# Attention scores in two matmul passes instead of three, with stacked query halves and doubled keys

## The chip, the cores and the metric

The kernel runs on one core of one Trainium2 chip. The metric is the device time of one execution in microseconds (us), lower is better. The engines are PE (TensorE), DVE (VectorE), ACT (ScalarE), POOL (GpSimd) and SP (SyncE, which here only issues transfers).

## The reference

Sliding-window attention with four sink tokens, then two mixer layers. Shapes: q, k, v are 2 x 8 x 768 x 64 in fp32; the model width is 512.

```python
scores = q @ k.T / sqrt(64)                # per batch and head
keep = (pos_k < 4) | ((pos_q - pos_k >= 0) & (pos_q - pos_k < 128))
a = softmax(where(keep, scores, -1e9))
x = concat_heads(a @ v)                    # 2 x 768 x 512

h = x.transpose(0, 2, 1) @ U @ V           # mixer 1, rank 32
u = x + h.transpose(0, 2, 1)
x = u + relu(u @ w_ch1) @ w_ch2            # 512 -> 2048 -> 512

h = relu(x.transpose(0, 2, 1) @ w_tok1) @ w_tok2    # mixer 2, 256
u = x + h.transpose(0, 2, 1)
out = u + relu(u @ w_ch1b) @ w_ch2b        # 512 -> 1536 -> 512
```

## The kernel before, in words

Every fp32 product is made of fp32r matmuls on operands that are split in a high part (a cast) and a low part (the value less its high part): high x high, high x low, low x high. So a score is three passes.

Attention works on 12 tiles of 128 queries (T = 0 to 5 are batch 0, T = 6 to 11 batch 1) and, inside a tile, on 8 heads; one head of one tile is a unit u = 8T + h. A head is 64 deep, so two heads (a pair) share the 128 contraction rows: q_hi and q_lo hold a pair in one 128 x 128 block, the even head in rows 0 to 63 and the odd one in rows 64 to 127. To keep the other head out, the key arrays k_hi and k_lo exist once for each head of the pair (index e) with zeros in the rows of the other head; they are set to zero once at the start. Each has three slots of 132 columns: 128 keys of a tile and 4 sink columns. A score matmul reads two slots, 264 columns, and runs over all 128 rows (L841 to L843).

The preparation of tile T + 1 happens during tile T: four PE transposes each for q and k into a bank (L827), an ACT copy out to q_full and k_full (L604, L611; both lie in the array uT_full), a DVE cast to the high part (q: L695, k: two casts of 64 rows, L711, and at T = 0 and 6 two small ones for the sinks, L710), and a POOL subtraction for the low part (q: L346, k: L357, in two steps of 64 rows). For T = 0 DVE does the subtractions. After the scores of a unit, DVE adds the mask and takes the maximum (L727), ACT makes the exponentials (L622), POOL copies the sink columns (L556), PE transposes them two units later (L850), ACT or DVE copies that out, and PE multiplies with v four units after the scores (L869). At the end of a tile (in unit h = 4 of the next one) DVE scales the result to x_nat (L749, L751, L754), and PE takes it in after unit h = 5 (the step "down", L887).

A hand-written list, plan, sets the order on every engine: each engine walks it and does its part of each step, in order, waiting on semaphores. attention(b) writes the units. Batch 0 is attention alone; the units of batch 1 are put one by one between the matmul steps of mixer 1 for batch 0; the rest is mixers alone. SP walks the same list and issues all loads on one queue: q and k of tile T + 2 when the k transposes of T are done, v of the next tile, weights four chunks deep. The helper functions keys, key_parts, query_low, key_low and keys_split and the steps "qsplit", "ksplit" and "scores" are what the change touches.

## Time and profile before

| | |
|---|---|
| median of 3 runs | 672.23 us (671.92 to 672.86) |
| profiled execution, span | 671.3 us |
| PE busy | 651.1 us, 97% |
| POOL busy | 372.9 us, 56% |
| ACT busy | 296.1 us, 44% |
| DVE busy | 204.9 us, 31% |
| share of the 16 DMA engines | 40.4% |

The span is one execution in the profiler, from its first to its last instruction; the median is of other executions, and lies 0.9 us above the span (what is outside the span, and what differs between executions; the profile doesn't part them). Busy shares are means over stages that have different limits: batch 0 of the attention (the first 75 us or so), attention and mixer 1 interleaved (83 to 250 us), and mixers alone. To be read are the stages, the waits of PE in each, and the order in time around the places that the change touches.

### The profile page before, as it was taken

To read this page: it belongs to the slowest core of one execution; us is meant where nothing else is said; L and a number is where in the kernel's file an instruction comes from. 1 tells how busy PE (TensorE), PEld (TensorE's weight loads), DVE (VectorE), ACT (ScalarE), POOL (GpSimd) and SP (SyncE) were. 2 spreads that over 40 slices of the span, in tenths; PEclk is the share of its full clock that TensorE was granted. 3 is DMA by queue.
4 is the path that set the end of the run, shared out by engine and by line. 5 is a ranking of instruction groups with operands and counts; after the bars stand their busy time and mean duration, and the time that the engine had idled before them with its cause. 6 is when DMAs were issued, how large, how long until landed. Compare 5 with 4: busy or idle time off the path is not lost.

```text
span 671.3 us, 10346 instructions
## 1 busy us (share of the span) xinstructions
PE 651.1 (97%) x3652; PEld 587.5 (88%) x3652; DVE 204.9 (31%) x526; ACT 296.1 (44%) x693; POOL 372.9 (56%) x393
## 2 busy tenths in 40 slices
PE   6889999999999999999999999999999999999998
PEld 5878798989999899899999988999999989999996
DVE  7776552333353331231121123111311134012112
ACT  4656565445464444373333324333433347233331
POOL 8544466646555545545665653666666654566562
PEclk9999899999999999999999999999999999999999
DMA  8334254352323333424445442544444442444541
GB/s 182 90 80 111 48 142 125 97 133 79 103 83 91 95 83 106 122 77 116 126 126 172 125 126 59 160 126 127 116 124 128 123 123 80 117 128 126 163 125 63
DMA packets 119955, 76.00 MB, mean 113 GB/s; under 512 B 43968, under 2 KB 103872, under 8 KB 119904
## 3 DMA queue, kind: packets, MB, share of 16 engines
q1 hardware_dynamic: 119904, 75.34, 40.4%
q8 instruction: 30, 0.49, 0.3%
q14 instruction: 21, 0.17, 0.1%
HBM read 71.91 MB, written 3.15 MB: 112 GB/s over the span
## 4 chain that ended last, share of the span: by engine, by line
PE 91%; DVE 4%; issue 2%; ACT 1%; POOL 1%; DMA 0%; DVEq 0%; ACTq 0%; POOLq 0%
PE bank L959 35%; PE bank L984 35%; PE bank L842 4%; PE bank L869 4%; PE bank L850 3%; PE bank L943 3%; PE bank L906 2%; PE bank L887 2%; PE bank L827 1%; PE bank L924 1%; PE bank L980 1%; DVE k_hi L711 1%; DVE masked L727 1%; DVE x_nat L754 1%; DVE sums_eps L749 1%
## 5 line engine op out<-in xcount | busy, mean ns | idle before, releaser
L575 POOL TENSOR_TENSOR w_lo<-w_raw,w_hi 128x512 fp32r<-128x512 f32 (+1 forms) x238 | 301.8, 1286 | 202.1 <-ACT w_hi L596 201.7
L672 DVE SCALAR_TENSOR_TENSOR hid_lo<-bank,hid_hi 128x384 fp32r<-128x384 f32 x112 | 62.4, 558 | 351.9 <-ACT hid_hi L584 351.9
L584 ACT ACTIVATE hid_hi<-bank 128x384 fp32r<-128x384 f32 x112 | 55.0, 491 | 246.5 <-PE bank L959 246.4
L959 PE MATMUL bank<-uT_hi,w_hi 128*128 128x384 f32 x448 | 153.1, 342 | 0.0
L959 PE MATMUL bank<-uT_hi,w_lo 128*128 128x384 f32 x448 | 151.1, 337 | 0.0
L959 PE MATMUL bank<-uT_lo,w_hi 128*128 128x384 f32 x448 | 150.6, 336 | 0.0
L596 ACT ACTIVATE w_hi<-w_raw 128x512 fp32r<-128x512 f32 (+1 forms) x238 | 138.1, 618 | 1.2 <-PE bank L906 1.2
L984 PE MATMUL bank<-w_hi,hid_hi 128*128 128x512 f32 x336 | 134.1, 399 | 0.0
L984 PE MATMUL bank<-w_hi,hid_lo 128*128 128x512 f32 x336 | 132.7, 395 | 0.0
L984 PE MATMUL bank<-w_lo,hid_hi 128*128 128x512 f32 x336 | 132.3, 394 | 0.0
L959 PEld LDWEIGHTS bank<-uT_hi,w_hi 128*128 128x128 f32 x448 | 84.3, 188 | 3.7 <-DVE uT_lo L675 0.2
L959 PEld LDWEIGHTS bank<-uT_lo,w_hi 128*128 128x128 f32 x448 | 84.2, 188 | 3.5
L959 PEld LDWEIGHTS bank<-uT_hi,w_lo 128*128 128x128 f32 x448 | 84.1, 188 | 0.0
L622 ACT ACTIVATE probs<-masked,neg_max 128x264 f32<-128x264 f32 x96 | 49.5, 516 | 74.7 <-DVE neg_max L727 74.2
L984 PEld LDWEIGHTS bank<-w_hi,hid_lo 128*128 128x128 f32 x336 | 63.0, 188 | 13.8
L984 PEld LDWEIGHTS bank<-w_lo,hid_hi 128*128 128x128 f32 x336 | 63.3, 188 | 10.4
L984 PEld LDWEIGHTS bank<-w_hi,hid_hi 128*128 128x128 f32 x336 | 63.3, 188 | 9.6
L556 POOL COPY p_sink<-probs 128x12 f32<-128x12 f32 x96 | 19.0, 200 | 71.2 <-ACT probs L622 69.7
L727 DVE CUSTOM_DVE_ANT_0 masked<-bank,masks 128x264 f32<-128x264 f32 x96 | 41.2, 430 | 40.7 <-PE bank L842 36.8
L869 PE MATMUL bank<-v_nat,probs_T 128*128 128x64 f32 x352 | 50.2, 261 | 0.8 <-DVE probs_T L738 0.4
L869 PEld LDWEIGHTS bank<-v_nat,probs_T 128*128 128x128 f32 x352 | 48.2, 191 | 2.3 <-ACT probs_T L630 1.2
L850 PE MATMUL bank<-ident,probs 128*128 128x128 f32 x176 | 36.2, 280 | 3.9 <-DVE p_sinkT L743 1.7
(82 smaller groups left out, 628.5 us busy)
## 6 DMA issues: line engine op xcount, KB each, us to landing
w_raw<-in_moe_w_ch_dram SPq DMA_DIRECT2D x224, 256.0 KB, 2.8
q_nat<-in_q_dram SPq DMA_DIRECT2D x12, 256.0 KB, 3.0
k_nat<-in_k_dram SPq DMA_DIRECT2D x12, 256.0 KB, 3.6
v_nat<-in_v_dram SPq DMA_DIRECT2D x12, 256.0 KB, 3.2
out_dram<-o_stage SPq DMA_DIRECT2D x12, 256.0 KB, 3.3
w_raw<-in_moe_w_tok_dram SPq DMA_DIRECT2D x6, 256.0 KB, 2.9
w_raw<-in_moe_w_tok_dram SPq DMA_DIRECT2D x8, 192.0 KB, 2.3
U_sb<-in_moe_U_dram SPq DMA_DIRECT2D x3, 96.0 KB, 3.3
```

The source lines that it names most:

```text
L575: nc.gpsimd.tensor_tensor(w_lo[:, split % NW, 0:n], w_raw[:, split % NR, 0:n], w_hi[:, split % NW, 0:n].bitcast(f32), ALU.subtract) \
L584: nc.scalar.activation(dst, m_tile(key)[0:rows, 0:dst.shape[-1]], func).then_inc(hi_ready, 1)
L596: nc.scalar.activation(w_hi[:, split % NW, 0:n], w_raw[:, split % NR, 0:n], ACT.Copy) \
L622: nc.scalar.activation(probs[:, u % 4, :], masked[:, u % 3, :], ACT.Exp, bias=neg_max[:, u % (2 * H):u % (2 * H) + 1], scale=-1.0, accum_o ...
L672: nc.vector.scalar_tensor_tensor(out=dst, in0=src, scalar=0.0, in1=hi.bitcast(f32), op0=ALU.max, op1=ALU.subtract).then_inc(m_drained, 1)
L727: nc.vector.tensor_tensor_reduce(out=masked[:, u % 3, :], in0=s_slots(u)[0][:, 0:NK], in1=masks[:, mask_of(T), :], scale=1.0, scalar=3.0e3 ...
L842: last = mm(bank[:, 0:NK], qs[:, T % 2, h // 2, :], keys(ks, T, h // 2, h % 2), start=(n == 0), stop=(n == 2))
L850: last = nc.tensor.transpose(tp_banks[tp_bank_of[s]][:, j * P:(j + 1) * P], probs[:, u % 4, col:col + P], ident[:, :])
L869: last = mm(o_bank(T)[:, h * D:(h + 1) * D], probs_T[:, u % 2, j * P:(j + 1) * P], v_nat[:, tile % 3, h * D:(h + 1) * D], start=(h == 0 an ...
L943: last = mm(m_tile(use)[:, 0:HALF], tok[:, g, rows], w[:, slot, 0:HALF], start=False, stop=(g == KG - 1 and n == 2), skip_group_check=True)
L959: last = mm(m_tile(use)[:, 0:HALF], w[:, slot, rows], u[:, kk, cols], start=(n == 0), stop=(n == 3 * KD - 1))
L984: last = mm(m_tile(use)[:, :], hid[:, hid_slot(s), toks], w[:, slot, :], start=False, stop=(final and n == 2), skip_group_check=True)
```

## The change

The two scores passes that share the keys' high part become one: for the even head the 128 contraction rows now hold the high part of q in rows 0 to 63 and its low part in rows 64 to 127, and the keys' high part stands in both halves. One pass over it gives high x high + low x high. The second pass has the keys' low part in both halves, and gives high x low and, new, low x low. The odd head is the mirror of this. q_hi and q_lo become one array q_st (index e for the head of the pair); q_lo and the new key_lo are scratch places in uT_full.

Since engines work lane by lane, a low part that was made in rows 0 to 63 comes to rows 64 to 127 by a DMA within the chip. For each tile there are 2 such copies for q and 6 for k, of 64 partitions x 4 x 512 B (128 KB) each; at T = 0 and T = 6 four more for the sinks, 64 partitions x 12 x 16 B each. T = 0 issues them on ACT's queue, the others on SP's, at a new step "stack" that the plan puts at unit h = 4 (for T = 6 behind the last unit of batch 0). PE's first scores of a tile wait for all of them (q_stacked, k_stacked). The casts on DVE now write both copies at once (128 x 1024 where 128 x 512 and 2 x 64 x 512 were), POOL's low part of k is one step of 128 rows where two of 64 rows were. The steps move too: the k transposes and the split of q in batch 0 from h = 2 to h = 1, the split of k from h = 4 and h = 6 to h = 2. Only slot 2 of the key arrays is set to zero at the start.

```diff
             if u == 0:
-                now += [("qT", T), ("kT", T), ("qsplit", T), ("ksplit", T)]
+                now += [("qT", T), ("kT", T), ("qsplit", T), ("ksplit", T), ("stack", T)]
             if lo <= u - LAG_V < hi and (u - LAG_V) % H == H - 1:
                 now.append(("sinksT", (u - LAG_V) // H))
             if u == hi and T < NTILES:
                 now.append(("ksplit", T))
             if u == hi + 1 and T < NTILES:
-                now.append(("ksplit_odd", T))
+                now.append(("stack", T))
             if u < hi and T + 1 < NTILES:
                 if h == 0:
                     now.append(("qT", T + 1))
-                if h == (2, 1)[b]:
+                if h == 1:
                     now += [("kT", T + 1), ("qsplit", T + 1)]
+                if h == 2 and T + 1 < hi // H:
+                    now.append(("ksplit", T + 1))
                 if h == 4 and T + 1 < hi // H:
-                    now.append(("ksplit", T + 1))
-                if h == 6 and T + 1 < hi // H:
-                    now.append(("ksplit_odd", T + 1))
+                    now.append(("stack", T + 1))
...
-        q_hi = sb("q_hi", [P, 2, PAIRS, P], f32r)
-        q_lo = sb("q_lo", [P, 2, PAIRS, P], f32r)
-        k_hi = sb("k_hi", [P, PAIRS, 2, 3, BLK], f32r)
-        k_lo = sb("k_lo", [P, PAIRS, 2, 3, BLK], f32r)
+        q_st = sb("q_st", [P, 2, 2, PAIRS, P], f32r)
+        k_hi = sb("k_hi", [P, 2, PAIRS, 3, BLK], f32r)
+        k_lo = sb("k_lo", [P, 2, PAIRS, 3, BLK], f32r)
...
+        q_lo = uT_full[:, :, 2 * P:3 * P].bitcast(f32r)
+        key_lo = uT_full[:, :, 3 * P:4 * P].bitcast(f32r)
...
+            eng.tensor_tensor(q_lo[:, :, :], q_full, q_st[:, T % 2, 0, :, :].bitcast(f32),
+                              ALU.subtract).then_inc(q_split, 1)
...
+        def key_low_parts(eng, T):
+            eng.tensor_tensor(key_lo[:, :, :], k_full, k_hi[:, 0, :, T % 3, 0:P].bitcast(f32),
+                              ALU.subtract).then_inc(k_split, 1)
+            if T % NQ == 0:
+                for e in range(2):
+                    eng.tensor_tensor(sink_columns(k_lo, e), sink_source(), sink_columns(k_hi, e).bitcast(f32),
+                                      ALU.subtract).then_inc(k_split, 1)
...
+        def stack_queries(queue, T):
+            queue.wait_ge(q_split, T + 1)
+            for rows, other, e in ((TOP, LOW, 0), (LOW, TOP, 1)):
+                queue.dma_start(q_st[other, T % 2, e, :, :].bitcast(f32), q_lo[rows, :, :].bitcast(f32)) \
+                     .then_inc(q_stacked[T % 2], 16)
+        def stack_keys(queue, T):
+            queue.wait_ge(k_split, keys_split(T))
+            slot, done = T % 3, k_stacked[T % 2]
+            for rows, other, e in ((TOP, LOW, 0), (LOW, TOP, 1)):
+                queue.dma_start(k_hi[other, e, :, slot, 0:P].bitcast(f32), k_hi[rows, e, :, slot, 0:P].bitcast(f32)) \
+                     .then_inc(done, 16)
+                for to in (rows, other):
+                    queue.dma_start(k_lo[to, e, :, slot, 0:P].bitcast(f32), key_lo[rows, :, :].bitcast(f32)) \
+                         .then_inc(done, 16)
+                if T % NQ == 0:
+                    for k_pad in (k_hi, k_lo):
+                        queue.dma_start(sink_columns(k_pad, e)[other].rearrange("p a s k -> p (a s) k").bitcast(f32),
+                                        sink_columns(k_pad, e)[rows].rearrange("p a s k -> p (a s) k").bitcast(f32)).then_inc(done, 16)
...
+                elif s[0] == "stack" and s[1]:
+                    stack_queries(sp, s[1])
+                    stack_keys(sp, s[1])
...
-                    pool.wait_ge(q_high, s[1] + 1)
-                    query_low(nc.gpsimd, s[1])
-                elif s[0] in ("ksplit", "ksplit_odd") and s[1]:
-                    pool.wait_ge(k_high, s[1] + 1)
-                    pool.wait_ge(psink_ready, copied)
-                    pool.wait_ge(q_split, s[1] + 1)
-                    if split:
-                        pool.wait_ge(wlo_ready, split)
-                    key_low(nc.gpsimd, pool.wait_ge, s[1], int(s[0] == "ksplit_odd"))
+                    T = s[1]
+                    pool.wait_ge(q_high, T + 1)
+                    pool.wait_ge(q_stacked[(T - 1) % 2], 32 * ((T - 1) // 2 + 1))
+                    query_low(nc.gpsimd, T)
+                elif s[0] == "ksplit" and s[1]:
+                    T = s[1]
+                    pool.wait_ge(k_high, T + 1)
+                    pool.wait_ge(k_stacked[(T - 1) % 2], keys_stacked(T - 1))
+                    key_low_parts(nc.gpsimd, T)
...
+                if s == ("stack", 0):
+                    stack_queries(nc.scalar, 0)
+                    stack_keys(nc.scalar, 0)
...
-                    nc.vector.tensor_copy(q_hi[:, T % 2, :, :], q_full).then_inc(q_high, 1)
+                    nc.vector.tensor_copy(q_st[:, T % 2, :, :, :], q_full.unsqueeze(1).broadcast_to([P, 2, PAIRS, P])) \
+                      .then_inc(q_high, 1)
...
-                    for src, dst, sinks, sink_dst in key_parts(k_hi, T):
-                        if T % NQ == 0:
-                            nc.vector.tensor_copy(sink_dst, sinks)
-                        last = nc.vector.tensor_copy(dst, src)
-                    last.then_inc(k_high, 1)
+                    if T % NQ == 0:
+                        for e in range(2):
+                            nc.vector.tensor_copy(sink_columns(k_hi, e), sink_source())
+                    nc.vector.tensor_copy(k_hi[:, :, :, T % 3, 0:P],
+                                          k_full.unsqueeze(1).broadcast_to([P, 2, PAIRS, P])).then_inc(k_high, 1)
...
-                        pe.wait_ge(q_split, T + 1)
-                        pe.wait_ge(k_split, keys_split(T) - (2 if T % NQ == 0 else 1))
-                    elif h == 1:
-                        pe.wait_ge(k_split, keys_split(T))
+                        pe.wait_ge(q_stacked[T % 2], 32 * (T // 2 + 1))
+                        pe.wait_ge(k_stacked[T % 2], keys_stacked(T))
                     bank, n = s_slots(u)
                     if u >= n:
                         pe.wait_ge(masked_ready, u - n + 1)
-                    for n, (qs, ks) in enumerate(((q_hi, k_hi), (q_hi, k_lo), (q_lo, k_hi))):
-                        last = mm(bank[:, 0:NK], qs[:, T % 2, h // 2, :], keys(ks, T, h // 2, h % 2),
-                                  start=(n == 0), stop=(n == 2))
+                    for n, ks in enumerate((k_hi, k_lo)):
+                        last = mm(bank[:, 0:NK], q_st[:, T % 2, h % 2, h // 2, :], keys(ks, T, h // 2, h % 2),
+                                  start=(n == 0), stop=(n == 1))
```

How the order moves on SP, from the 12th of its rows on (loads of tiles 2 and 3, then of tile 4). Before:

```order
L431 DMA q_nat<-in_q_dram 128x8x64
L433 DMA k_nat<-in_k_dram 128x8x64
L431 DMA q_nat<-in_q_dram 128x8x64
L433 DMA k_nat<-in_k_dram 128x8x64
L439 DMA v_nat<-in_v_dram 128x8x64
```

With the change:

```order
L462 DMA q_nat<-in_q_dram 128x8x64
L464 DMA k_nat<-in_k_dram 128x8x64
L378 DMA q_st<-uT_full 64x4x128 x2
L386 DMA k_hi<-k_hi 64x4x128
L389 DMA k_lo<-uT_full 64x4x128 x2
L386 DMA k_hi<-k_hi 64x4x128
L389 DMA k_lo<-uT_full 64x4x128 x2
```

The eight copies of a tile stand behind the loads of q and k (for two tiles on) in the same queue, and ahead of the load of v.

On ACT at the start of the program, with the change (q_full and k_full are in uT_full; before, nothing stood between the second copy-out and the third):

```order
L646 ACTIVATE uT_full<-bank0 128x4x128 [waits tp_ready]
L378 DMA q_st<-uT_full 64x4x128 [waits q_split]
L378 DMA q_st<-uT_full 64x4x128
L386 DMA k_hi<-k_hi 64x4x128 [waits k_split]
L389 DMA k_lo<-uT_full 64x4x128 x2
L393 DMA k_hi<-k_hi 64x12x4
L393 DMA k_lo<-k_lo 64x12x4
L386 DMA k_hi<-k_hi 64x4x128
L389 DMA k_lo<-uT_full 64x4x128 x2
L393 DMA k_hi<-k_hi 64x12x4
L393 DMA k_lo<-k_lo 64x12x4
L639 ACTIVATE uT_full<-bank4 128x4x128 [waits tp_ready,q_split]
```

ACT's own work for tile 1 now stands behind twelve issues, ten of which wait for the last subtraction of tile 0.

On DVE in a tile of batch 0, from unit h = 1 to the end of tile work in unit h = 4 (L727 and L762 are the masks, two rows each). Before:

```order
L695 CAST q_hi<-uT_full 128x512
L727 ISA masked,neg_max<-bank,masks 128x264
L727 ISA neg_max 128x1
L738 COPY probs_T<-bank 128x256
L743 TENSOR_TENSOR p_sinkT<-bank,p_sinkT 32x128
L727 ISA masked,neg_max<-bank,masks 128x264
L727 ISA neg_max 128x1
L711 CAST k_hi<-uT_full 64x4x128 x2
L727 ISA masked,neg_max<-bank,masks 128x264
L727 ISA neg_max 128x1
L749 TENSOR_SCALAR sums_eps<-sums 128x8
```

With the change:

```order
L730 CAST q_st<-uT_full 128x1024
L762 ISA masked,neg_max<-bank,masks 128x264
L762 ISA neg_max 128x1
L747 CAST k_hi<-uT_full 128x8x128
L762 ISA masked,neg_max<-bank,masks 128x264
L762 ISA neg_max 128x1
L773 COPY probs_T<-bank 128x256
L778 TENSOR_TENSOR p_sinkT<-bank,p_sinkT 32x128
L762 ISA masked,neg_max<-bank,masks 128x264
L762 ISA neg_max 128x1
L762 ISA masked,neg_max<-bank,masks 128x264
L762 ISA neg_max 128x1
```

The casts of k leave the place right ahead of the tile's end work (L749), and stand one unit behind the cast of q.

## Rows read from the trace of the kernel before

**Rows 1.** The page: busy time by engine, chain that ended last.
```profile
PE 651.1 (97%) x3652; PEld 587.5 (88%) x3652; DVE 204.9 (31%) x526; ACT 296.1 (44%) x693; POOL 372.9 (56%) x393
...
PE 91%; DVE 4%; issue 2%; ACT 1%; POOL 1%; DMA 0%; DVEq 0%; ACTq 0%; POOLq 0%
```

**Rows 2.** Stretch of batch 1: length, busy PE, PEld, DVE, ACT, POOL, PEclk, DMA, GB/s.
```profile
83.00:250.00 167.00, 163.94 (x1011) 151.27 (x1010) 62.32 (x192) 85.78 (x222) 97.41 (x117) 1.00 0.37 103
```

**Rows 3.** Timeline of PE, one unit: start, duration, line, names.
```profile
41.21 0.37 PE L842 MATMUL bank<-k_hi,q_hi 128*128 128x264 f32 x1
41.41 0.29 PE L842 MATMUL bank<-k_lo,q_hi 128*128 128x264 f32 x1
41.54 0.28 PE L842 MATMUL bank<-k_hi,q_lo 128*128 128x264 f32 x1
41.66 0.56 PE L869 MATMUL bank<-v_nat,probs_T 128*128 128x64 f32 x4
```

**Rows 4.** Timeline around the end of tile work, in tiles 2 and 5.
```profile
34.66 1.27 POOL L357 TENSOR_TENSOR k_lo<-uT_full,k_hi 64x512 fp32r<-64x512 f32 x1
...
34.79 1.18 DVE L749 TENSOR_SCALAR sums_eps<-sums 128x8 f32<-128x8 f32 x1
...
36.98 1.10 PE L887 MATMUL bank<-x_nat,U_sb 128*96 128x512 f32 x2 [1.35 <-DVE x_nat L754]
...
70.36 0.17 DVE L749 TENSOR_SCALAR sums_eps<-sums 128x8 f32<-128x8 f32 x1
```

**Rows 5.** Timeline of the program's start, up to the first scores.
```profile
5.97 0.60 ACT L611 ACTIVATE uT_full<-bank 128x512 f32<-128x512 f32 x1 [0.26 <-PE bank L827]
...
6.31 0.69 DVE L346 TENSOR_TENSOR q_lo<-uT_full,q_hi 128x512 fp32r<-128x512 f32 x1
...
7.99 1.78 DVE L357 TENSOR_TENSOR k_lo<-uT_full,k_hi 64x48 fp32r<-64x48 f32 x4
...
9.07 0.56 PE L842 MATMUL bank<-k_hi,q_hi 128*128 128x264 f32 x1 [0.93 <-DVE k_lo L357]
```

**Rows 6.** SP's queue: issues in time (start, duration, tile, count).
```profile
3.83 1.08 SPq L433 DMA_DIRECT2D k_nat<-in_k_dram  x1
...
8.49 1.85 SPq L469 DMA_DIRECT2D U_sb<-in_moe_U_dram  x3
...
10.38 1.26 SPq L473 DMA_DIRECT2D o_stage<-o_stage  x2
...
42.91 0.37 SPq L431 DMA_DIRECT2D q_nat<-in_q_dram  x1
```

**Rows 7.** The page's DMA issues: count, KB of each, median us to landing.
```profile
w_raw<-in_moe_w_tok_dram SPq DMA_DIRECT2D x8, 192.0 KB, 2.3
...
o_stage<-o_stage SPq DMA_DIRECT2D x2, 128.0 KB, 3.1
```

**Rows 8.** Groups by form: count, busy us, mean ns, idle before.
```profile
L357 POOL TENSOR_TENSOR k_lo<-uT_full,k_hi 64x512 fp32r<-64x512 f32 x22 | 28.4, 1291 | 7.7 <-DVE k_hi L711 4.2 <-POOL w_lo L575 1.5 <-POOL p_sink L556 0.3
...
L682 DVE CAST v_sink<-o_stage 96x1024 fp32r<-96x1024 f32 x1 | 0.7, 726 | 0.0
L710 DVE CAST k_hi<-uT_full 64x48 fp32r<-64x48 f32 x4 | 0.7, 179 | 0.0
L357 POOL TENSOR_TENSOR k_lo<-uT_full,k_hi 64x48 fp32r<-64x48 f32 x2 | 0.5, 268 | 0.3 <-POOL k_lo L357 0.2
```

**Rows 9.** Timeline of PE: first scores of tiles 1 and 5, last unit of 5, first of 6.
```profile
17.11 0.37 PE L842 MATMUL bank<-k_hi,q_hi 128*128 128x264 f32 x1
...
64.71 0.37 PE L842 MATMUL bank<-k_hi,q_hi 128*128 128x264 f32 x1
...
73.40 0.37 PE L842 MATMUL bank<-k_hi,q_hi 128*128 128x264 f32 x1
...
83.82 0.37 PE L842 MATMUL bank<-k_hi,q_hi 128*128 128x264 f32 x1
```

**Rows 10.** Timeline of DVE: last cast of the keys of tile 6.
```profile
75.03 0.42 DVE L711 CAST k_hi<-uT_full 64x512 fp32r<-64x512 f32 x1
```

More of the change, by code:

```diff
@@ L287, in attention_then_two_mixers @@
         k_split = sem("k_split")
+        q_stacked = [sem(f"q_stacked{i}") for i in range(2)]
+        k_stacked = [sem(f"k_stacked{i}") for i in range(2)]
         probsT_by_act = sem("probsT_by_act")
@@ L344, in query_low @@
         def query_low(eng, T):
-            eng.tensor_tensor(q_lo[:, T % 2, :, :], q_full,
-                              q_hi[:, T % 2, :, :].bitcast(f32), ALU.subtract).then_inc(q_split, 1)
-        def key_low(eng, wait, T, e):
-            low, high = list(key_parts(k_lo, T))[e], list(key_parts(k_hi, T))[e]
-            steps = ((3, 2), (1, 0)) if T % NQ == 0 else ((1, 0),)
-            done = (keys_split(T - 1) if T else 0) + e * len(steps)
-            for to, of in steps:
-                wait(k_split, done)
-                eng.tensor_tensor(low[to], low[of], high[to].bitcast(f32), ALU.subtract).then_inc(k_split, 1)
-                done += 1
-            wait(k_split, done)
@@ L361, in keys_split, with sink_columns, sink_source @@
-        def keys_split(T):
-            return sum(4 if t % NQ == 0 else 2 for t in range(T + 1))
+            eng.tensor_tensor(q_lo[:, :, :], q_full, q_st[:, T % 2, 0, :, :].bitcast(f32),
+                              ALU.subtract).then_inc(q_split, 1)
+        def sink_columns(k_pad, e):
+            return k_pad[:, e, :, :, P:BLK]
+        def sink_source():
+            return k_full[:, :, 0:N_SINK].unsqueeze(2).broadcast_to([P, PAIRS, 3, N_SINK])
+        def key_low_parts(eng, T):
[5 more added lines that the diff above has]
+                                      ALU.subtract).then_inc(k_split, 1)
@@ new lines, in keys_split, with key_moves, keys_stacked @@
+        def keys_split(T):
+            return sum(3 if t % NQ == 0 else 1 for t in range(T + 1))
+        def key_moves(T):
+            return 10 if T % NQ == 0 else 6
+        def keys_stacked(T):
+            return sum(16 * key_moves(t) for t in range(T % 2, T + 1, 2))
+        def stack_queries(queue, T):
[3 more added lines that the diff above has]
+                     .then_inc(q_stacked[T % 2], 16)
@@ L663, in _ @@
         def _(dve):
[L664 to L666 removed]
+            nc.vector.memset(k_hi[:, :, :, 2, :].rearrange("p a b k -> p (a b) k").bitcast(f32), 0.0) \
+              .then_inc(khi_zeroed, 1)
             def low_of(key, rows, dst, hi, relu=False):
```

39 lines of the change are left out of this document (14 added, 25 removed).

## The prediction

> **What bounds the kernel now.** I read the page first, then the stretches, then the waits and the order in time on PE. The page shows PE busy 97% of the span and 91% of the chain that ended last [rows 1]: what leaves PE's stream is gained, where PE really is the last to come. In the stretch of batch 1 it is: PE is busy 163.9 of 167 us there, and the DMA engines at 0.37 [rows 2]. In batch 0 it is so inside a tile: the three score matmuls follow one another without a gap [rows 3]; but once a tile PE waits 1.35 us for x_nat [rows 4]. Before 9.07 us PE has nothing to multiply: the scores of tile 0 wait for its splits [rows 5]. So there are three stages with three limits, and the change touches each in another way.
>
> **What the pass is worth.** In a unit the second pass starts 0.20 us after the first, the third 0.13 us after it, and the next work 0.12 us after that [rows 3]. The third one goes: 0.12 us for each of 96 units. The 48 units of batch 1 give 48 x 0.12 = 5.8 us, since PE is full there and a tile's copies have the time of four units spread over mixer steps. Tile 5, whose successor's copies don't stand between its own units, gives 8 x 0.12 = 1.0 us.
>
> **What the copies cost by themselves.** No row shows a 64-row copy within the chip. The nearest is the copy o_stage<-o_stage: on-chip, also 128 KB, two of them issued in 1.26 us, so 0.63 us each [rows 6], and landed 3.1 us after the issue [rows 7]. The low end is a queue with nothing in the way, 0.37 us for an issue [rows 6] and 2.3 us to landing (192 KB, rows 7); the high end a queue full of loads, 1.08 us for an issue [rows 6]. I take 0.63 and 3.1, the same kind and size.
>
> **The start, tile 0.** The q cast becomes 1024 columns wide; the row of a 1024-column cast says 0.73 us [rows 8]. The cast in use takes 0.2 us less, so the subtraction of q ends at 6.31 + 0.69 + 0.2 = 7.2 us [rows 5]. Behind it on DVE: two sink casts of 0.18, the k cast of 0.73, the subtraction of 0.69, two small ones of about 0.26 each [rows 5, 8]. That is 9.5 us, where it now ends at 9.77 [rows 5]: DVE gains a little. But then ten copies are issued on ACT: the last at 9.5 + 9 x 0.63 = 15.2, landed at 18.3. First scores at 18.3 and not 9.07: **+9.2 us**. Nothing covers this, the whole program waits. ACT's work for tile 1 stands behind these issues too, but PE, DVE and POOL would have nothing for it to feed. Ends: 9.5 + 9 x 0.37 + 2.3 = 15.1 (+6.0), and 9.5 + 9 x 1.08 + 3.1 = 22.3 (+13.2).
>
> The four sink copies move 16 B at a time, 768 pieces each. The nearest row is the load of U, three issues in 1.85 us, 0.62 each [rows 6]; I charge them like the rest. The Trainium skill (DMA: Bandwidth & Descriptors, "Why small descriptors are slow (HBM only)") says that copies inside SBUF don't pay the small-piece penalty; by that they would cost no more than an empty issue, and the sum would be about 1 us smaller here and 1 us at tile 6. No row shows it.
>
> **Tiles 1 to 5, from the first scores of one to those of the next.** Now PE sets the pace: tile 0 takes 17.11 - 9.07 = 8.0 us, the four periods from tile 1 to tile 5 take 64.71 - 17.11 = 47.6 us [rows 9], 11.9 each. With the change a chain runs from the first scores of tile T to those of T + 1: k transposes done about 1.4 us after the first scores (they now follow unit 0), ACT's copy 0.6 [rows 5] and its queue, to 2.2; DVE's cast 0.73 behind a mask, to 3.1; POOL 1.29 [rows 8], to about 4.5. Then six copies: last issue 4.5 + 5 x 0.63 = 7.65, landed at 10.75. The two copies of q fit before it (3.1 to 4.4). So the period can't be under about 10.7 us. PE alone would need less: 11.9 - 8 x 0.12 = 10.9, and the wait of 1.35 us goes too: the two k casts of 0.42 us [rows 10] no longer stand ahead of L749, and L749 itself took 1.18 us while POOL's subtraction of k ran beside it and 0.17 us in tile 5, where none did; there PE had no wait [rows 4]. That leaves 9.6. The copies end last, and PE waits 1.1 us at each tile's start. **Tile 0's period: 10.7 against 8.0, +2.7. The four others: 42.8 against 47.6, -4.8.** The moved casts come at the price of 1.5 us of DVE work in two neighbouring units; the transposes have two units of slack, so I cost that at nothing while PE has a wait at the tile's end to give.
>
> Here a rule speaks against the change. L749 in rows 4 shows a DVE instruction that lasted until POOL's ended. The Trainium skill (SBUF — State Buffer, "Who interferes with whom") states why: a copy, cast or tensor_scalar in a two-port mode and a GpSimd instruction exclude each other for their whole length. By it the k cast, now one unit behind q's, would wait for POOL's subtraction of q.
>
> Priced from rows: POOL starts that subtraction after the q cast, at 1.7, ends at 3.0, and the k cast would start there and not at 2.4. That is 0.6 us on five chains, +3.0; I leave it out of the sum, because no row shows a cast waiting, and keep it in the range.
>
> **Tile 6.** Its sink columns overwrite those in use, so its casts wait for the last scores of batch 0. They now end at 75.45 [rows 10]; with the wide cast the same. POOL: a start 0.3 later, 1.29 and 2 x 0.27 [rows 8] give 77.5. Ten copies: last issue 83.2, landed 86.3. PE comes to these scores at 83.82 [rows 9], all on the old time base: **+2.5**. Ends: nothing (77.5 + 3.3 + 2.3 = 83.1), and 77.5 + 9.7 + 3.1 = 90.3 (+6.5).
>
> Elsewhere: two 0.9 us zeroings go from the start of DVE and POOL, which had time there; POOL loses 1.29 us of work a tile and is not the bound; SP's waits for the splits hold back weight loads by less than the chunks that are ahead. All nothing.
>
> **The sum.** +9.2 + 2.7 - 4.8 - 1.0 + 2.5 - 5.8 = +2.8 us on a span of 671.3; the median lies 0.9 us above that span, and I carry this over: 672.2 + 2.8 = **675.0 us**. About 1.3 us, 0.2%, is what a measurement of this kernel can tell from no change, so this is slower, by little.
>
> **The rivals.**
> *The copies hide (ends on the other side: faster).* If an issue costs 0.37 and a landing 2.3 us, as in the empty stretches, the chain is 4.5 + 1.9 + 2.3 = 8.7 us, under PE's 9.6. Then +6.0 at the start, +0.7 for tile 0's period, 4 x (9.6 - 11.9) = -9.2, nothing at tile 6, -1.0 - 5.8: -9.3, 662.9 us. It decides where the sum falls under nothing, at a chain of about 10.1 us with the start at +9.2. For it: SP's queue is nearly empty in batch 0 apart from q and k. Against it: these loads are issued 1.5 us ahead of the copies, in the same queue.
> *The queue is full.* With 1.08 us an issue, the last of eight copies from 3.1 on is issued at 10.7 and landed at 13.8: +13.2 at the start, +5.8, 4 x 1.9 = +7.6, +6.5, -1.0 - 5.8: +26, 698 us. For it: 1 MB of copies a tile beside 768 KB of loads.
> *The small sink pieces are dear.* If the four cost 2 us each rather than 0.63, tile 0 and tile 6 are each 5.5 us later: 686 us.
> *DVE sets the pace in batch 0*, by the wait of the casts or by the two wide casts in a row: the forecast's five chains 0.6 to 1 us longer, 678 to 680 us.
> *The pass is worth nothing* because PE's stream is paced by others in batch 1: speaks against it that PE is 98% busy there. It would give 681 us.
>
> **Chances.** Forecast 0.42; hidden copies 0.26; full queue 0.11; dear sinks 0.08; DVE 0.10; no worth 0.03. The forecast's own range, 668 to 680, holds a little of both other signs. Faster by over 0.2%: 0.25 from hidden copies and 0.09 from the forecast: 0.34. Within 0.2%: 0.12. Slower: 0.54. The range reaches from the hidden copies to the dear sinks, 662 to 688, and leaves out the full queue and some of the ends.
>
> **What would show it.** First scores at about 18 us, idle PE before them, released by a DMA into k_lo or k_hi; PE waits of about 1 us for such a DMA at the first scores of tiles 1 to 5, and of 2 to 3 us at tile 6; issues of q_st, k_hi, k_lo spaced 0.6 us; L749 at 0.2 us and no wait for x_nat in batch 0; the stretch of batch 1 shorter by 6 us. I am wrong if the start costs under 7 or over 12 us, if PE waits for DVE or ACT and not for DMA in batch 0, or if the periods lie outside 10 to 11.5 us.

## The result, and the profile after

The changed kernel takes 687.56 us (median of 4 runs, 686.87 to 689.26) against 672.08 us before; the ratio is 1.023, with a 95% interval of 1.022 to 1.025. That is 15.5 us slower where I had forecast 2.8 us slower. The profiled execution has a span of 686.0 us against 671.3, so 14.7 us more, and all stages below are of these two. Executions of one kernel differ in PE's mean granted clock, and in time with it: the four of the changed kernel had spans of 685.1 us (mean granted clock 0.998) to 687.5 (0.988).

The page of the changed kernel, the lines that answer to [rows 1], and its queues:

```profile
PE 644.4 (94%) x3556; PEld 577.7 (84%) x3556; DVE 204.8 (30%) x512; ACT 296.2 (43%) x693; POOL 359.7 (52%) x381
...
PE 87%; DVE 4%; issue 4%; ACT 2%; DMA 1%; ACTq 1%; DVEq 0%
...
q1 hardware_dynamic: 146976, 86.93, 47.9%
q10 hardware_dynamic: 5312, 1.10, 1.0%
```

PE has 96 matmuls fewer and is busy 6.7 us less; but its share of the chain fell from 91% to 87%. Queue q10 is new: the copies that ACT issues.

The timeline of PE in the changed kernel, at the first scores of tiles 0 to 6. They answer to [rows 5, 9]; in brackets is how long PE had been idle. "issue" as a releaser here is a wait that the profile couldn't put down to an instruction; by time and by the program it is the copies' semaphore.

```profile
22.06 0.56 PE L875 MATMUL bank<-k_hi,q_st 128*128 128x264 f32 x1 [13.86 <-DMA k_lo<-k_lo]
33.41 0.56 PE L875 MATMUL bank<-k_hi,q_st 128*128 128x264 f32 x1 [3.29 <-issue]
45.43 0.36 PE L875 MATMUL bank<-k_hi,q_st 128*128 128x264 f32 x1 [0.58 <-issue]
56.91 0.36 PE L875 MATMUL bank<-k_hi,q_st 128*128 128x264 f32 x1 [0.61 <-issue]
68.73 0.37 PE L875 MATMUL bank<-k_hi,q_st 128*128 128x264 f32 x1
80.47 0.36 PE L875 MATMUL bank<-k_hi,q_st 128*128 128x264 f32 x1 [0.85 <-issue]
100.78 0.36 PE L875 MATMUL bank<-k_hi,q_st 128*128 128x264 f32 x1 [2.69 <-issue]
```

Cut at these starts, the 14.7 us stand so (the last scores are those of unit 95, at 264.56 us against 249.65 us):

| stretch | before | after | change | forecast |
|---|---|---|---|---|
| to the first scores | 9.07 | 22.06 | +13.0 | +9.2 |
| tile 0's period | 8.04 | 11.35 | +3.3 | +2.7 |
| tile 1 to tile 5 | 47.60 | 47.06 | -0.5 | -4.8 |
| tile 5 to tile 6 | 19.11 | 20.31 | +1.2 | +1.5 |
| first to last scores of batch 1 | 165.83 | 163.78 | -2.1 | -5.8 |
| the rest | 421.65 | 421.44 | -0.2 | 0 |

Three rows are off: the start by 3.8 us, tiles 1 to 5 by 4.3, batch 1 by 3.7. They are 11.8 of the 11.9 us by which the sum was too small.

The fourth row, tile 5 to tile 6, agrees only by luck. In the profiled execution of the kernel before, PE ran at half clock there for about 3 us:

```profile
79.00:82.00 3.00, 3.00 (x9) 1.81 (x10) 0.44 (x1) 1.07 (x3) 0.01 (x1) 0.50 0.00 0
```

```profile
78.87 2.02 PE L887 MATMUL bank<-x_nat,U_sb 128*96 128x512 f32 x2 [0.85 <-DVE x_nat L754]
```

(The row of the stretch has the columns of [rows 2]; 0.50 is the granted clock.) The same two matmuls take 1.10 us in the changed kernel. e10_split_late, which has the kernel before's order in this stretch and full clock, takes 17.83 us for it (63.77 to 81.60). Against that, the change costs 2.5 us here.

**The start.** The timeline of ACT's queue and of SP's, start and duration of each group of issues:

```profile
9.16 0.60 ACTq L386 DMA_DIRECT2D k_hi<-k_hi  x1
...
11.15 1.08 ACTq L393 DMA_DIRECT2D k_hi<-k_hi  x1
12.25 1.15 ACTq L393 DMA_DIRECT2D k_lo<-k_lo  x1
13.43 1.36 ACTq L386 DMA_DIRECT2D k_hi<-k_hi  x1
14.82 1.34 ACTq L389 DMA_DIRECT2D k_lo<-uT_full  x2
...
16.95 0.70 ACTq L393 DMA_DIRECT2D k_lo<-k_lo  x1
```

```profile
10.68 2.15 SPq L504 DMA_DIRECT2D o_stage<-o_stage  x2
12.88 1.12 SPq L462 DMA_DIRECT2D q_nat<-in_q_dram  x1
14.04 1.02 SPq L464 DMA_DIRECT2D k_nat<-in_k_dram  x1
```

The splits of tile 0 are ready at 9.16 us (forecast 9.5). The first three key copies are issued 0.6 to 0.7 us apart, as forecast; the next three, from 11.15 us on, while SP issues too, 1.1 to 1.4 us apart; the last four, from 14.82 on, again 0.7 apart. The last is issued at 16.95 and landed at 22.06. SP's own copy o_stage<-o_stage, 1.26 us for two before [rows 6], takes 2.15. The page's DMA issues (KB of each, median us to landing) show the same:

```profile
k_lo<-uT_full SPq DMA_DIRECT2D x44, 128.0 KB, 2.7
...
k_lo<-uT_full ACTq DMA_DIRECT2D x4, 128.0 KB, 5.4
...
o_stage<-o_stage SPq DMA_DIRECT2D x2, 128.0 KB, 5.5
...
k_hi<-k_hi SPq DMA_DIRECT2D x2, 12.0 KB, 2.4
```

**A tile of batch 0.** The period of tile 2, whose first scores are at 45.43 us and in which tile 3 is prepared, on DVE, POOL and SP:

```profile
46.91 0.68 DVE L730 CAST q_st<-uT_full 128x1024 fp32r<-128x1024 f32 x1
47.86 1.65 DVE L747 CAST k_hi<-uT_full 128x1024 fp32r<-128x1024 f32 x1
```

```profile
47.67 1.28 POOL L342 TENSOR_TENSOR uT_full<-uT_full,q_st 128x512 fp32r<-128x512 f32 x1
48.90 0.66 POOL L588 COPY p_sink<-probs 128x12 f32<-128x12 f32 x1
49.59 1.27 POOL L355 TENSOR_TENSOR uT_full<-uT_full,k_hi 128x512 fp32r<-128x512 f32 x1
```

```profile
50.88 0.59 SPq L386 DMA_DIRECT2D k_hi<-k_hi  x1
51.52 1.28 SPq L389 DMA_DIRECT2D k_lo<-uT_full  x2
52.84 0.62 SPq L386 DMA_DIRECT2D k_hi<-k_hi  x1
```

The wide cast takes 0.68 us where it starts ahead of POOL's work, and 1.65 us where POOL's subtraction of q runs already: it ends 0.6 us after that one. The split of k is done 5.4 us after the tile's first scores, not 4.5 (5.4 to 6.0 in the five periods). The hold isn't all of this: POOL itself is at the subtraction of q until 48.95 us and has a p_sink copy behind it (0.19 us alone, here 0.66), so with a cast that nobody holds it could have begun the subtraction of k at about 49.14 and not at 49.59. By that estimate the hold is 0.45 us of the delay and POOL's own queue the other 0.5. Then the copies are as forecast: 0.65 us apart, the last landed about 2.7 us after its issue, and tile 3's first scores start at 56.91 us, 11.5 us after tile 2's.

What this costs is less than it looks. At the first scores of tiles 2, 3 and 5 PE has waited 0.58, 0.61 and 0.85 us, and at tile 4's (68.73 us) not at all: 2.0 us in four periods.

**Batch 1.** Its start, on PE, DVE and POOL. The four matmuls L969 took 0.97 us before PE's wait for tile 6, and 1.63 us after it:

```profile
96.68 0.97 PE L969 MATMUL bank<-V_sb,low 96*128 96x384 f32 x4
...
103.15 1.63 PE L969 MATMUL bank<-V_sb,low 96*128 96x384 f32 x4
...
110.77 0.39 PE L875 MATMUL bank<-k_hi,q_st 128*128 128x264 f32 x1 [0.64 <-DVE neg_max L762]
```

```profile
109.33 1.03 DVE L747 CAST k_hi<-uT_full 128x1024 fp32r<-128x1024 f32 x1
```

```profile
108.53 1.28 POOL L607 TENSOR_TENSOR w_lo<-w_raw,w_hi 128x512 fp32r<-128x512 f32 x1
```

Two costs stand here that no term of mine had: the clock, and a k cast that is kept waiting by POOL's subtraction of a weight chunk (1.03 us and not 0.69), then the mask behind it, then PE (0.64 us). The granted clock shows the first. Here is the stretch behind the wait, and the same one in e9_tile0_free, where PE has waited 2.71 us at the same place and the clock stays full (columns as in [rows 2]):

```profile
101.00:104.00 3.00, 3.00 (x17) 3.00 (x17) 0.44 (x2) 0.75 (x3) 0.19 (x1) 0.58 0.00 0
```

```profile
91.00:94.00 3.00, 2.94 (x24) 2.72 (x23) 1.27 (x4) 1.97 (x6) 0.19 (x1) 1.00 0.00 0
```

The loss lies mostly in the first four units. From the first scores of batch 1 to those of its fifth unit, and from there to the last:

| run | first four units | the other 43 steps |
|---|---|---|
| before | 12.1 | 153.7 |
| e4_moves_only | 13.15 | 153.7 |
| e8_no_copies | 13.2 | 150.3 |
| after | 13.4 | 150.3 |
| e9_tile0_free | 12.4 | 150.3 |
| e3_third_pass | 14.4 | 154.2 |

Between the changed kernel and e9_tile0_free the first column differs by 1.06 us: I take that as the price of the half clock here, from one profiled execution of each. The second column prices the pass where nothing else changes: 3.4 us between before and after, 3.8 us between e3_third_pass and after, so 0.08 to 0.09 us each.

### The profile page after: what moved, and what is told of

It reads as the page before. It is cut to its first block, busy times and chain, and to the rows that moved or that the text cites. A ratio compares the mean times of both kernels' runs of the same rounds, so it can differ in the third digit from the quotient of the medians.

```text
span 686.0 us, 10179 instructions
## 1 busy us (share of the span) xinstructions
PE 644.4 (94%) x3556; PEld 577.7 (84%) x3556; DVE 204.8 (30%) x512; ACT 296.2 (43%) x693; POOL 359.7 (52%) x381
## 4 chain that ended last, share of the span: by engine, by line
PE 87%; DVE 4%; issue 4%; ACT 2%; DMA 1%; ACTq 1%; DVEq 0%
PE bank L1017 34%; PE bank L992 34%; PE bank L902 4%; PE bank L883 3%; PE bank L875 3%; PE bank L976 3%; PE bank L939 2%; PE bank L920 1%; PE bank L862 1%; PE bank L957 1%; DVE masked L762 1%; PE bank L1013 1%; DMA k_lo<-k_lo 1%; PE bank L911 1%; DVE q_st L730 0%
## 5 line engine op out<-in xcount | busy, mean ns | idle before, releaser
L588 POOL COPY p_sink<-probs 128x12 f32<-128x12 f32 x96 | 22.4, 233 | 98.8 <-ACT probs L657 96.6
L762 DVE CUSTOM_DVE_ANT_0 masked<-bank,masks 128x264 f32<-128x264 f32 x96 | 40.6, 428 | 57.1 <-PE bank L875 49.1
L875 PE MATMUL bank<-k_hi,q_st 128*128 128x264 f32 x96 | 35.7, 371 | 22.5 <-DMA k_lo<-k_lo 13.9
```

The lines of the kernel that those rows point to most:

```text
L588: nc.gpsimd.tensor_copy(p_sink[:, T % 2, :].rearrange("p (c n) -> p c n", c=3)[:, :, N_SINK * h:N_SINK * (h + 1)], probs[:, u % 4, P:BLK]. ...
L762: nc.vector.tensor_tensor_reduce(out=masked[:, u % 3, :], in0=s_slots(u)[0][:, 0:NK], in1=masks[:, mask_of(T), :], scale=1.0, scalar=3.0e3 ...
L875: last = mm(bank[:, 0:NK], q_st[:, T % 2, h % 2, h // 2, :], keys(ks, T, h // 2, h % 2), start=(n == 0), stop=(n == 1))
```

## The experiments

All are compared with the kernel before on the same chip; starts of tiles are read from each one's PE timeline. Line numbers differ between kernels by a few.

**Are the slow copies at the start the loads' doing?** (e1_hold)

```diff
+            sp.wait_ge(k_stacked[0], keys_stacked(0))
             load_v(1)
             for n in range(3):
                 sp.dma_start(U3_sb[:, :, n * RANK:(n + 1) * RANK],
```

> The changed kernel, but SP issues its loads of v for tile 1, of U and of q and k for tiles 2 and 3 only when the copies of tile 0 have landed. In the changed kernel the ten key copies of tile 0 take 8.5 us to issue on ACT (9.16 to 17.65 us) and land at 22.06. Theory A, these copies share the DMA engines with SP's loads: each issue falls to about 0.64 us as on SP later, the landing to 2.7, so first scores at 9.16 + 9 x 0.64 + 2.7 = 17.6 us, 4.4 us earlier, and the total 3 to 4.4 us lower. Theory B, the copies of tile 0 are slow by themselves (16-byte pieces, ACT's queue): first scores stay at 21 to 22 us, and the total stays or grows by the loads that now come later.

686.49 us, ratio 1.021 (1.020 to 1.023). The timeline of its ACT queue and of SP's:

```profile
15.26 0.71 ACTq L393 DMA_DIRECT2D k_lo<-k_lo  x1
```

```profile
17.56 0.40 SPq L470 DMA_DIRECT2D v_nat<-in_v_dram  x1
...
24.81 1.52 SPq L378 DMA_DIRECT2D q_st<-uT_full  x2
```

The ten copies are issued 0.6 to 0.7 us apart from 9.16 to 15.26 us. First scores at 17.68 us, against 17.6 expected: theory A for the copies, in that SP's loads beside them cost 4.4 us. Whether the two meet in the DMA engines or already where the transfers are issued, this run doesn't part. But the total fell by 1.1 us only, hardly clear of the spread of executions, where I expected 3 to 4.4: the loads now fill SP's queue up to 24.8 us, ahead of tile 1's copies, and tile 0's period is 14.7 us, not 11.35. The queue was only relieved in one place to be full in the next.

**Does POOL hold up DVE's cast?** (e2_qlo_dve)

```diff
-                elif s[0] == "qsplit" and s[1]:
+                elif s[0] == "qsplit" and s[1] >= NQ:
...
-                    if T == 0:
-                        dve.wait_ge(q_high, 1)
+                    if T < NQ:
+                        dve.wait_ge(q_high, T + 1)
+                        if T:
+                            dve.wait_ge(q_stacked[(T - 1) % 2], 32 * ((T - 1) // 2 + 1))
                         query_low(nc.vector, T)
```

> The changed kernel, but in batch 0 DVE makes q's low part (0.7 us) and not POOL (1.28 us). In the changed kernel DVE's cast of k lasts 1.65 us and ends when POOL's subtraction of q ends. Theory A, DVE's cast is kept waiting by POOL's instruction, and the chain cast, POOL subtraction, six copies sets the period of tiles 1 to 5: the cast falls to 0.7 us though 0.7 us of DVE work is put ahead of it, key copies start 0.3 to 0.9 us earlier after the tile's first scores, and the total falls by 1 to 4 us. Theory B, the cast is long because its broadcast source is slow: it stays at 1.65 us, all chains get 0.7 us longer, and the total grows by about 3 us.

687.86 us, ratio 1.023 (1.021 to 1.025). Its k cast (here L749) in the period of tile 2:

```profile
49.04 0.69 DVE L749 CAST k_hi<-uT_full 128x1024 fp32r<-128x1024 f32 x1
```

```profile
49.82 0.19 POOL L588 COPY p_sink<-probs 128x12 f32<-128x12 f32 x1 [1.73 <-ACT probs L657]
50.26 1.27 POOL L355 TENSOR_TENSOR uT_full<-uT_full,k_hi 128x512 fp32r<-128x512 f32 x1 [0.24 <-issue]
```

The cast is 0.69 us, so its source pattern isn't slow: in the changed kernel it waited for POOL. Theory A on the cause. On the time neither theory's number came: the chain isn't shorter. The subtraction put ahead on DVE takes 0.7 us, POOL starts the k subtraction 0.5 us after the cast instead of at once, behind a p_sink copy that waits for the exponentials, and the key copies start (at 51.56 us) 5.8 us after the tile's first scores at 45.77, where they started after 5.45. So what the hold alone costs in time isn't shown by this run.

**What is the pass worth where copies are waited for?** (e3_third_pass)

```diff
-                    for n, ks in enumerate((k_hi, k_lo)):
+                    for n, ks in enumerate((k_hi, k_lo, k_lo)):
                         last = mm(bank[:, 0:NK], q_st[:, T % 2, h % 2, h // 2, :], keys(ks, T, h // 2, h % 2),
-                                  start=(n == 0), stop=(n == 1))
+                                  start=(n == 0), stop=(n == 2))
```

> The changed kernel with a third pass put back in every unit, as a repeat of the pass over the keys' low part (the scores then hold that part twice). It prices the pass in the changed kernel. Theory A, PE waits for the copies in batch 0 and is the bound only from tile 6 on: the periods of tiles 0 to 4 stay within 0.2 us, batch 1 and tile 5 grow, in all +5 to +7 us. Theory B, PE still sets the pace everywhere: 96 x 0.12 = +11.5 us. Theory C, batch 1 isn't paced by PE either: under +3 us.

694.4 us, 6.8 us above the changed kernel: theory A. From the first to the last scores of batch 1 it is 168.6 us and not 163.8, 4.8 us for 48 passes, 0.10 us each; a part of this is a longer spell at half clock in its first units (0.55 from 104 to 109 us). Without the first four units it is 0.09. Tiles 0 to 3 take 47.7 us from the first scores (21.88 to 69.60) against 46.7, so their passes were nearly free. Tile 4 is a miss: its period is 13.4 us against 11.7. SP's queue shows why:

```profile
75.83 2.81 SPq L389 DMA_DIRECT2D k_lo<-uT_full  x2
```

Two issues that take 1.28 us elsewhere take 2.81 here, and PE waits 2.12 us for the copies; the half clock follows (0.66 from 84 to 89 us). This is the slowest of the run's four executions, 2.9 us above their median, so its stages add up to 9.2 us by the last scores and not to 6.8.

**What do the moved steps do alone?** (e4_moves_only)

```diff
-                if h == (2, 1)[b]:
+                if h == 1:
                     now += [("kT", T + 1), ("qsplit", T + 1)]
-                if h == 4 and T + 1 < hi // H:
+                if h == 2 and T + 1 < hi // H:
                     now.append(("ksplit", T + 1))
-                if h == 6 and T + 1 < hi // H:
+                if h == 3 and T + 1 < hi // H:
                     now.append(("ksplit_odd", T + 1))
```

> The kernel before, three passes and no copies, with the moved steps alone: k transposes and the split of q at unit h = 1, the two halves of the split of k at h = 2 and 3. Theory A, PE's wait of 1.35 us for x_nat in tiles 1 to 4 comes from the k casts and POOL's subtraction standing beside the tile's end work: the waits go, the total falls by 3 to 5.5 us, to about 667 to 669 us. Theory B, the wait moves: DVE's cast of k is now kept waiting by POOL's subtraction of q, the masks of h = 2 are late, PE waits for probs_T instead: the total stays within 1.3 us.

673.89 us, ratio 1.0026 (1.0016 to 1.0036): 1.8 us slower, a bit more than theory B said. Tiles 1 to 5 take 47.62 us against 47.60, so nothing was gained there; batch 1 takes 166.8 against 165.8. The casts of k in the period of its tile 2, on DVE, and what ran on POOL:

```profile
32.43 1.50 DVE L711 CAST k_hi<-uT_full 64x512 fp32r<-64x512 f32 x2
...
36.27 0.70 DVE L749 TENSOR_SCALAR sums_eps<-sums 128x8 f32<-128x8 f32 x1
```

```profile
31.93 1.28 POOL L346 TENSOR_TENSOR q_lo<-uT_full,q_hi 128x512 fp32r<-128x512 f32 x1
...
35.66 1.27 POOL L357 TENSOR_TENSOR k_lo<-uT_full,k_hi 64x512 fp32r<-64x512 f32 x1
```

Two casts that took 0.85 us take 1.50; sums_eps still takes 0.70. PE's waits for x_nat fell from 5.4 to 1.3 us by the table of waits, but waits for probs_T and neg_max took their place.

**Was the third pass cover for a copy out of the transposes' bank?** (e5_after_tail on the changed kernel, e6_before_tail on the one before)

```diff
-            now, scores, probsT, pv = [], [], [], []
+            now, scores, probsT, pv, tail = [], [], [], [], []
...
                 if h == 0:
-                    now.append(("qT", T + 1))
+                    (tail if b else now).append(("qT", T + 1))
...
-            now += scores + pv + probsT
+            now += scores + pv + probsT + tail
```

("kT" and "qsplit" move in the same way.)

> The changed kernel, but in batch 1 the q and k transposes of the next tile (and the split of q behind them) stand at the end of a unit, behind the transposes of the probabilities, and not at its head. The scores of batch 1 took 163.8 us from the first to the last in the changed kernel and 165.8 before: the 0.12 us of a pass give 5.6 us there, but only 2 came. Theory A, the pass was cover: the transposes of q or k and the next transposes of probabilities use one bank, and the two score passes between them are now too short for ACT's copy out of that bank (0.6 us), so PE waits 0.4 us where it waited less. With the order changed these waits go, batch 1 gets 2 to 4 us shorter, and so the total. Theory B, the gain is lost elsewhere (the clock after PE's long waits, masks that come late): the total stays within 1.3 us.

> The kernel before with the same move of the q and k transposes in batch 1 to the end of a unit. Three passes are the cover there; PE's weight loads for the transposes of probabilities still sat idle 4.0 us in 11 places. Theory A: most of that goes, total 2 to 4 us lower, about 669 us. Theory B, three passes are cover enough: within 1.3 us.

696.44 and 680.47 us: 8.9 and 7.6 us slower than their base, on the wrong side of both theories. The table of waits of e6_before_tail, PE:

```profile
PE bank L827 <- ACT probs_T L630: 5.8, 4, 1.8
...
PE bank L827 <- DVE probs_T L738: 2.7, 4, 1.0
```

At the end of a unit the q and k transposes stand right behind the probabilities' in the same bank, and wait for a copy-out that itself stands behind other work on ACT and DVE. I had looked at who follows the transposes in the bank and not at who goes before. So the question wasn't tested, and stays open.

**Is it the half of the rows that limits a copy?** (e7_alternate)

```diff
-            for rows, other, e in ((TOP, LOW, 0), (LOW, TOP, 1)):
+            halves = ((TOP, LOW, 0), (LOW, TOP, 1))
+            for rows, other, e in halves:
                 queue.dma_start(k_hi[other, e, :, slot, 0:P].bitcast(f32), k_hi[rows, e, :, slot, 0:P].bitcast(f32)) \
                      .then_inc(done, 16)
-                for to in (rows, other):
-                    queue.dma_start(k_lo[to, e, :, slot, 0:P].bitcast(f32), key_lo[rows, :, :].bitcast(f32)) \
+            for cross in (True, False):
+                for rows, other, e in halves:
+                    queue.dma_start(k_lo[other if cross else rows, e, :, slot, 0:P].bitcast(f32), key_lo[rows, :, :].bitcast(f32)) \
                          .then_inc(done, 16)
...
```

> The changed kernel with the same copies in another order: k's copies alternate between reading rows 0 to 63 and reading rows 64 to 127, where three in a row read the same half. In the changed kernel each is issued 0.64 us after the last, 205 GB/s. Theory A, the rate is that of one half's ports, and copies in opposite directions overlap: the spacing falls to 0.35 to 0.5 us, each chain by 0.5 to 1.2 us, the start by 1 to 2, the total by 4 to 8 us. Theory B, the rate is that of the engines or of the queue whatever the half: spacing 0.6 to 0.65, total within 1.3 us.

687.54 us, ratio 1.021 (1.019 to 1.024), the changed kernel's time. SP's queue:

```profile
50.57 1.25 SPq L387 DMA_DIRECT2D k_hi<-k_hi  x2
51.87 2.62 SPq L391 DMA_DIRECT2D k_lo<-uT_full  x4
```

0.63 and 0.66 us a copy, whichever half is read next: theory B. The spacing isn't helped by directions in one queue.

**What if copies were free?** (e8_no_copies)

```diff
         def stack_queries(queue, T):
-            queue.wait_ge(q_split, T + 1)
+            return
...
         def stack_keys(queue, T):
-            queue.wait_ge(k_split, keys_split(T))
+            return
...
-                        pe.wait_ge(q_stacked[T % 2], 32 * (T // 2 + 1))
-                        pe.wait_ge(k_stacked[T % 2], keys_stacked(T))
+                        pe.wait_ge(q_split, T + 1)
+                        pe.wait_ge(k_split, keys_split(T))
```

(The waits of POOL and ACT for copies change likewise, and the whole of k_lo is set to zero at the start.)

> The changed kernel without any of its on-chip copies and without the waits for them; casts, subtractions, moved steps and two passes stay, the keys' low array is set to zero once. The scores thus lack the low parts. It shows what the change would bring if copies were free. Theory A, copies are the whole loss: first scores at 9.3 us, tile 0 to tile 1 8 us, tiles 1 to 5 with PE as the bound 9.6 to 10.7 us each, nothing waited for at tile 6, in all 661 to 666 us. Theory B, the moved steps and wide casts cost on their own (moves alone made the kernel before 1.8 us slower): 667 to 671 us.

667.9 us, ratio 0.992 (0.989 to 0.995): theory B's range. The copies thus cost about 20 us in all, and two passes with everything else of the change gain 4.9 us and not the 11.5 us of 96 passes at 0.12. By stretches against before: start +0.4, tile 0 -0.2, tiles 1 to 5 -2.7 (44.9 us), tile 5 to 6 -1.6 (17.52 us; 1.3 of it is the half clock of the kernel before), batch 1 -2.3 (163.5 us). Batch 1 is as long as with the copies (163.8), so **the copies alone don't explain its small gain**: without them its first four units are as slow as in e4_moves_only (13.2 and 13.15 us against 12.1 before), and with them the half clock behind the wait costs.

**Is the start a cost of its own?** (e9_tile0_free)

```diff
         def stack_keys(queue, T):
+            if T == 0:
+                return
```

(the same for the queries, and the waits for tile 0's copies go to its splits)

> The changed kernel without the copies of tile 0 alone, and without the waits for them; all other copies stay. The scores that read tile 0's keys or queries lack parts. Theory A, the start is a cost of its own, +13.0 us at the first scores, and little of it comes back later: the total falls by 12 to 14 us, to 673 to 676 us. Theory B, the queue is what is short: SP's loads and the copies of tile 1 must pass it anyway, tile 1 becomes late in place of tile 0, and the total falls by under 9 us.

677.33 us, ratio 1.008 (1.006 to 1.009): 10.2 us less than the changed kernel, between the theories. First scores are at 9.45, 12.6 us earlier; tile 1's at 23.14, 10.3 us earlier; about 1 us of the total is batch 1's clock, which stayed full in the profiled execution. SP's queue:

```profile
15.38 1.77 SPq L380 DMA_DIRECT2D q_st<-uT_full  x2
```

Tile 1's copies stand behind the loads up to 15.4 us, as in e1_hold: 2.3 us of the start come back there.

**Can the wait for x_nat be had by order alone?** (e10_split_late, on the kernel before)

```diff
-                if h == 4 and T + 1 < hi // H:
+                if h == 5 and T + 1 < hi // H:
                     now.append(("ksplit", T + 1))
```

> The kernel before (three passes, no copies), with only the split of k moved, from h = 4 and 6 to h = 5 and 6, behind the tile's end work. PE's wait of 1.35 us for x_nat in tiles 1 to 4 of the kernel before is put down to two things that stand ahead of or beside the end work on DVE: the k casts (0.85 us) and POOL's subtraction, which keeps the instruction sums_eps for 1.18 us. Theory A, this is so, and it can be moved away from: sums_eps takes 0.2 us, the waits for x_nat go, and the total falls by 3 to 5.5 us, to 667 to 669 us. Theory B, as in the run with the moves alone, POOL's work meets another DVE instruction or PE meets the k split of the next tile: the total stays within 1.3 us or grows.

670.21 us, ratio 0.9963 (0.9948 to 0.9978): 2.6 us faster than before, the only full kernel here that beats it. The instruction sums_eps over the whole program (min, median, max in ns):

```profile
L749 DVE TENSOR_SCALAR sums_eps<-sums x12: 159/164/216, 23.8 to 260.4; 128x8 f32<-128x8 f32 x12
```

Theory A on the mechanism: no sums_eps is kept waiting, and PE's waits for x_nat fall from 5.4 to 0.9 us by the table of waits. The total misses its range: it fell by 2.6 us where 3 was the least. A part even of this may be the clock: executions with a mean granted clock of 1.00 take 669.6 us here and 671.8 before, which is 2.2 us. New waits for probs_T (1.8 us) take a part of the gain.

## Why the prediction was wrong, point by point

*What bounds the kernel.* Right for batch 0's start. In batch 1 it holds from the fifth unit on; in the first four the late casts and the clock decide.

*The start, +9.2.* It measured +13.0. The splits (9.16 us) and the undisturbed issue (0.6 us) were right. The step that failed is "I take 0.63 and 3.1", used as if ACT's ten copies had the chip's transfers to themselves. The end that I had priced with a full queue, +13.2, is what came, though not quite in that way: only three issues took over 1 us, and the landing of the last took 5.1 us. e1_hold shows that SP's loads made it so. I had the row of SP's queue in hand, which is issuing from 0.74 to 15 us.

*Small sink pieces, charged like the rest.* Right: 12 KB in pieces of 16 B took 0.62 to 0.68 us of SP's queue, as much as 128 KB in pieces of 512 B, and landed in 2.4 us against 2.7. They also keep the DMA engines busy. At tile 6 of the changed kernel, first a stretch with mostly sink copies on their way (issued at 94.38 and 95.05 us), then one with copies of 128 KB (issued from 96.47 on; columns as in [rows 2]; the last two are the busy share of the DMA engines and GB/s):

```profile
96.00:97.00 1.00, 0.91 (x8) 0.67 (x7) 0.63 (x1) 1.00 (x3) 0.49 (x1) 1.00 0.60 21
98.00:99.00 1.00, 0.09 (x1) 0.00 (x0) 1.00 (x3) 1.00 (x4) 1.00 (x2) 1.00 0.91 183
```

A ninth of the bytes, for two thirds of the busy time. The rule that I quoted from the Trainium skill (DMA: Bandwidth & Descriptors, "Why small descriptors are slow (HBM only)") doesn't hold here for copies inside SBUF; the measurement decides.

*Tiles 1 to 5, -4.8.* It measured -0.5. Two steps failed, and they are told apart by e8_no_copies, where the stretch takes 44.9 us. One half of the miss, 2.2 us of 4.3, is the chain of the copies, 11.5 us and more where I had 10.7: the spacing and the landing (0.65, 2.7) were right, the split of k was late by 0.9 to 1.5 us. I had left out the hold of POOL on DVE's cast "because no row shows a cast waiting", and priced it at 0.6 us a tile. The hold is there: the Trainium skill (SBUF — State Buffer, "Who interferes with whom") had it, the trace agrees, 1.65 us against 0.69 in e2_qlo_dve, and I had the same thing in L749's 1.18 us [rows 4]. By the estimate above it is about half of the lateness; POOL's own subtraction of q, which ends 3.5 us after the first scores where my chain had the subtraction of k begin after 3.1, is the rest. e2_qlo_dve took the hold away and gained nothing, so the hold's price in time is argued and not shown.

*PE's own need, 9.6 us a tile.* This is the other half, 2.1 us. Without copies tiles 1 to 5 still take 11.2 us each. The passes gain 0.085 us each there (e8_no_copies against e4_moves_only), not 0.12. And the waits for x_nat, which I had as 1.35 us in each of the four periods (they are 0.55, 1.35, 1.34 and 1.33), do go, but the moved steps alone gain nothing (e4_moves_only): waits for probs_T and neg_max take their place. "I cost that at nothing" was the step that failed.

*Tile 6, +1.5 with tile 5.* It measured +1.2, but against a kernel before that ran at half clock there; the 83.82 us in my sum have that spell in them. Against e10_split_late it is +2.5: the copies cost 2.8 us (20.31 against 17.52 in e8_no_copies), with PE idle for 2.69 us, and the missing passes of tile 5 gained 0.3 and not 1.0. The number was luck.

*Batch 1, -5.8.* It measured -2.1. Of the 3.7 us between, 1.9 are in the units after the fourth: they gained 3.4 us, where 0.12 us a pass would give 5.3. Here the term was mis-sized: putting a pass back costs 0.09 us (e3_third_pass), not the 0.12 us read off one unit of batch 0; the last 0.5 us are not explained. The other 1.8 are in the first four units, 13.4 us where 12.1 less four passes was forecast. About 1.1 of them are the half clock behind the wait at tile 6, by the comparison with e9_tile0_free. The rest fits the late mask behind a held cast: the third unit takes 3.2 us against 2.6 before, and 3.4 to 3.5 in e4_moves_only, e8_no_copies and e9_tile0_free.

*The rivals.* None was it whole. The full queue had the start's number and nothing else. DVE's hold is seen in the tiles, but PE didn't lose by it what that rival said. The dear sinks' 686 us lies next to the result by luck: each such copy took 0.62 to 0.68 us on SP, not 2. Two of my own signs of being wrong came: a start of over 12 us, and periods outside 10 to 11.5 us (12.0, 11.8 and 11.7 of the four). And batch 1, which was to be shorter by 6 us, was by 2.

## What to carry to other kernels

Price a transfer with the traffic of the moment at which it is issued: here the same copy landed in 2.7 us and in 5.4, and the queue that was relieved at one place was full at the next. When an edit moves casts and subtractions, write down what stands beside them on DVE and on POOL: each lengthened the other's instructions here, and a chain through both engines is as long as the two queues make it. A wait that goes is not a gain until the next instruction to be late is named: the waits for x_nat went, and the tiles took as long as before. A pass taken off the busiest engine is worth its time only where that engine is the last to come: of 11.5 us of passes, 4.9 could be had even with free copies. And before a stretch of two profiles is compared, look at the granted clock of both in it: one row of my table agreed only because the kernel before ran at half clock there.

## What the runs showed of the hardware

- An on-chip copy of 64 partitions took 0.62 to 0.66 us of its queue for 128 KB, in either order of directions, and 0.62 to 0.68 us for 12 KB in 768 pieces. With a second queue busy, three issues in a row took 1.1 to 1.4 us, and the landing went from 2.7 to 5.4 us.
- A DVE cast that began behind a running POOL subtraction took 1.65 us and not 0.69; POOL's p_sink copy beside it took 0.66 us and not 0.19.
- The granted clock fell to 0.50, the lower of its two levels (1.2 and 2.4 GHz), behind PE's wait of 3.29 us (34 to 36 us) and behind that of 2.69 us (102 to 104), where L969 took 1.63 us against 0.97. But in e9_tile0_free it stayed at 1.00 behind a wait of 2.71 us at the same place, and in the kernel before it was 0.50 from 79 to 82 us behind a wait of only 0.85 us. So the length of the wait right before it doesn't decide it in these runs; the half clock cost about 1.1 us in batch 1 of the changed kernel.
